# A fused attention, gated convolution and feed-forward kernel: operand addresses, the first loads, blank matmuls, and an engine for wval's low parts

## The reference

```python
# attention, B=2, H=8, S=768, D=64; n_global=8, n_local=96
keep  = is_global | ((rel >= 0) & (rel < n_local))
s     = q @ k.T / sqrt(D) - slope[h] * dist          # masked where not keep
x     = softmax(s) @ v                               # then heads side by side: (2, 768, 512)
# block 1
gate  = sigmoid(causal_conv5(x, moe_conv_w))
x     = (gate * (x @ w_val)) @ w_out
# block 2
h     = relu(x @ w_in)                               # (2, 768, 1024)
gate  = sigmoid(conv3(h, moe2_conv_w))
out   = (h * gate) @ w_out2
```

## Time and profile before

| what | us |
|---|---|
| median of three runs (281.39 to 281.93) | 281.39 |
| the profiled execution | 282.07 |
| its span | 280.3 |
| TensorE busy | 268.7 |
| VectorE busy | 187.3 |
| ScalarE busy | 158.8 |
| GpSimd busy | 41.0 |

### The profile page before, as it was taken

The page is one execution under the profiler, slowest core; times in us unless marked ns, Lnnn a source line. Parts: engine busy times, 40 slices in busy tenths (PEclk is TensorE's granted clock), DMA queues, the critical chain, the costliest instruction groups (busy, mean ns, idle before and its releaser), DMA issues.

```text
span 280.3 us, 4450 instructions
## 1 busy us (share of the span) xinstructions
PE 268.7 (96%) x1552; PEld 207.3 (74%) x1552; DVE 187.3 (67%) x452; ACT 158.8 (57%) x362; POOL 41.0 (15%) x67
## 2 busy tenths in 40 slices
PE   2999999999999999999999999999999999997995
PEld 1444458888788888888888888888888888776884
DVE  0794367788899992698960896688603578999200
ACT  1132659889999991754543506675334466874410
POOL 1081016867233220000000000000000000000000
PEclk9999999999999999999999999999999999999999
DMA  6999715545672000000000000000021000000321
GB/s 206 368 346 301 284 37 150 154 127 182 189 223 75 4 0 2 5 0 2 0 0 0 2 0 0 0 2 1 0 103 49 0 0 0 1 2 0 150 78 72
DMA packets 11864, 21.83 MB, mean 78 GB/s; under 512 B 1728, under 2 KB 1728, under 8 KB 11712
## 3 DMA queue, kind: packets, MB, share of 16 engines
q1 hardware_dynamic: 11408, 21.50, 23.8%
q10 hardware_dynamic: 432, 0.02, 0.1%
HBM read 18.37 MB, written 3.15 MB: 77 GB/s over the span
## 4 chain that ended last, share of the span: by engine, by line
PE 79%; DVE 12%; ACT 5%; DMA 1%; issue 1%; SPq 0%
PE ps L516 16%; PE ps L518 16%; PE ps L517 16%; PE ps L416 11%; PE ps L487 6%; PE ps L447 6%; PE ps L465 6%; DVE hgB L1082 4%; ACT prob L652 3%; DVE hgA L1082 2%; PE ps L473 2%; DVE hglA L1095 2%; DMA win<-in_win 1%; DVE hgA L1089 1%; DVE hgB L1089 1%
## 5 line engine op out<-in xcount | busy, mean ns | idle before, releaser
L652 ACT ACTIVATE prob<-prob,low 128x256 f32<-128x256 f32 (+1 forms) x96 | 46.0, 486 | 4.4 <-DVE low L902 4.4
L518 PE MATMUL ps<-gh,Wl 128*128 128x512 f32 x96 | 38.3, 399 | 0.0
L517 PE MATMUL ps<-gl,Wh 128*128 128x512 f32 x96 | 37.9, 394 | 0.0
L516 PE MATMUL ps<-gh,Wh 128*128 128x512 f32 x96 | 37.7, 392 | 0.0
L766 ACT ACTIVATE h<-ps 128x512 f32<-128x512 f32 x24 | 14.4, 598 | 39.8 <-PE ps L518 39.6
L416 PE MATMUL ps<-win,w1t 128*128 128x512 f32 x64 | 31.0, 646 | 5.2 <-DMA win<-in_win 5.2
L1082 DVE SCALAR_TENSOR_TENSOR hgA<-h,cw,hgA 128x512 f32<-128x512 f32 x32 | 21.9, 746 | 20.1 <-ACT hgA L778 20.1
L927 DVE SCALAR_TENSOR_TENSOR g<-xT,cw,g 128x512 f32<-128x512 f32 x48 | 32.8, 746 | 2.2 <-ACT g L691 2.2
L902 DVE CUSTOM_DVE_ANT_0 prob<-ps,bias 128x256 f32<-128x256 f32 x80 | 30.0, 413 | 2.6 <-PE ps L447 2.6
L416 PEld LDWEIGHTS ps<-win,w1t 128*128 128x128 f32 x64 | 13.1, 207 | 21.6 <-issue 16.2
L516 PE MATMUL ps<-hghA,w2h 128*128 128x512 f32 x64 | 25.2, 393 | 0.7 <-DVE hglA L1095 0.7
(11 more groups left out here) (87 smaller groups left out, 502.4 us busy)
## 6 DMA issues: line engine op xcount, KB each, us to landing
q_rows<-in_q SPq DMA_DIRECT2D x12, 256.0 KB, 4.6
kW<-in_k SPq DMA_DIRECT2D x12, 256.0 KB, 4.6
v_own<-in_v SPq DMA_DIRECT2D x12, 256.0 KB, 3.1
out<-xT SPq DMA_DIRECT2D x5, 512.0 KB, 2.8
w<-in_w SPq DMA_DIRECT2D x8, 256.0 KB, 11.7
v_win<-in_v SPq DMA_DIRECT2D x10, 192.0 KB, 3.1
w1t<-in_w1t SPq DMA_DIRECT2D x4, 256.0 KB, 4.4
win<-in_win SPq DMA_DIRECT2D x4, 256.0 KB, 5.2
```

Of the source, the lines that this page charges most:

```text
L516: pe.matmul(out, w_hi, x_hi, start=first, stop=False)
L517: pe.matmul(out, w_hi, x_lo, start=False, stop=False)
L518: return pe.matmul(out, w_lo, x_hi, start=False, stop=final)
L652: act.activation(part, part, ACT.Exp, scale=-1.0, bias=low[:, t % 2, i:i + 1], accum_out=total[:, t % 2, i:i + 1]).then_inc(exp_done, 1)
```

## The change

It has five parts.

- Two pads are declared: 192 bytes after `nval` (with the new `blank`, 512 bytes) and 160 bytes after `h`. All operands that stood 64 bytes past a multiple of 256, and `gh` and `gl`, now begin at a multiple of 256.
- VectorE fills `blank` with zeros as its first instruction, and TensorE runs seven float32 matmuls of `blank` by `blank` (128 columns) into a bank that is overwritten later.
- Part m = 0 of W's first half is cut in two quarters of 256 columns (`first_part_W`). The first call waits for 64 KB of `w1t` and 128 KB of `win` alone (`start_in[0]`).
- The slices of `win` for the first half of W are issued by ScalarE, save the first quarter, and `nw` is ScalarE's fourth issue instead of its first; SP issues the `w1t` slices, `wval` and the second half of `win`.
- `wval_low` moves from POOL to VectorE, between the bias tables and the first `split_W`.

```diff
+        blank = sb("blank", [P, P])
...
+        sb("to_256_bytes", [P, 48])
...
         h = sb("h", [P, FT, B * HROW + 1])
+        sb("h_to_256_bytes", [P, 40])
...
         def _(sp):
-            for m in range(CT):
+            sp.dma_start(win[:, 0, 0:F // 4], A_win[:, 0, 0:F // 4]).then_inc(start_in[0], 16)
+            sp.dma_start(w1t[:, 0, P:C], A_w1t[:, 0, P:C]).then_inc(start_in[1], 16)
+            for m in range(1, CT):
                 sp.dma_start(w1t[:, m, :], A_w1t[:, m, :]).then_inc(w1_in[m], 16)
-                sp.dma_start(win[:, m, 0:F // 2], A_win[:, m, 0:F // 2]).then_inc(w1_in[m], 16)
...
-                wval_low()
-                pool.wait_ge(wvl_done, CT)
                 for t in range(3):
                     key_window(t)
...
-            for m in range(CT):
+            pe.wait_ge(blank_set, 1)
+            for _ in range(WARM):
+                pe.matmul(WB(2 * CT - 1)[:, 0:P], blank[:, :], blank[:, :], start=True, stop=True)
+
+            def first_part_W(k, quarter):
+                cols = slice(quarter * (F // 4), (quarter + 1) * (F // 4))
+                pe.matmul(WB(k)[:, cols], w1t[:, 0, k * P:(k + 1) * P], win[:, 0, cols], start=(quarter == 0), stop=False)
+
+            pe.wait_ge(start_in[0], 32)
+            first_part_W(0, 0)
+            pe.wait_ge(start_in[1], 16)
+            for k in range(1, CT):
+                first_part_W(k, 0)
+            pe.wait_ge(start_in[2], 16)
+            for k in range(CT):
+                first_part_W(k, 1)
+            for m in range(1, CT):
                 pe.wait_ge(w1_in[m], 32)
...
         def _(act):
-            act.dma_start(nw[:, :], A_n.partition_broadcast(P)).then_inc(n_in, 16)
+            act.dma_start(w1t[:, 0, 0:P], A_w1t[:, 0, 0:P]).then_inc(start_in[0], 16)
+            act.dma_start(win[:, 0, F // 4:F // 2], A_win[:, 0, F // 4:F // 2]).then_inc(start_in[2], 16)
+            for m in range(1, CT):
+                act.dma_start(win[:, m, 0:F // 2], A_win[:, m, 0:F // 2]).then_inc(w1_in[m], 16)
+                if m == 1:
+                    act.dma_start(nw[:, :], A_n.partition_broadcast(P)).then_inc(n_in, 16)
...
+            def wval_low():
+                for k in range(CT):
+                    dve.wait_ge(wvh_done, k + 1)
+                    dve.tensor_tensor(wvl[:, k, :], wval[:, k, :], wvh[:, k, :].bitcast(f32), ALU.subtract).then_inc(wvl_done, 1)
+
+            dve.memset(blank[:, :], 0.0).then_inc(blank_set, 1)
...
+                wval_low()
                 for i in range(CT + 2):
                     split_W(i)
```

More of the change, by code:

```diff
@@ L23 @@
 RING = 4
+WARM = 7
 PAIRS = H // 2
@@ L173, in program @@
         k_in, q_in, v_in = ([sem(f"{name}_in{slot}") for slot in range(RING)] for name in "kqv")
-        k_window = sem("k_window")
+        k_window, blank_set = sem("k_window"), sem("blank_set")
+        start_in = [sem(f"start_in{part}") for part in range(3)]
         consts, iotas, setup = sem("consts"), sem("iotas"), sem("setup")
@@ L338, in _ @@
             pool.memset(xT[:, :, :, 0:PAD1], 0.0).then_inc(x_edges, 1)
[L341 to L344, removed]
             def key_window(t):
```

## The result

The changed kernel takes 277.13 us (median of 6 executions, 276.42 to 278.13), the kernel before 281.60 beside it: a ratio of 0.9848, 95% interval 0.9829 to 0.9866, or 4.3 us less (3.8 to 4.8). Run again later, it took 277.17 with a ratio of 0.9863. The forecast was 277.0. The profiled execution took 277.47 with a span of 275.7, 4.6 less than before.

The account below looks back on a forecast made before the run. TensorE was taken as the bound, busy 96% of the span with 79% of the chain. Head -2.6 and `hid` -1.8 make -4.4 from 281.39, so 277.0 us; own range 275.7 to 278.7, eight in ten 269.9 to 279.8.

Parts of the forecast that it names:

- Head: Start of TensorE's work up to `qk(0)`: blank matmuls and smaller first slices bring real work and clock rise earlier, 2.6 us gained.
- The time from first work to the rise: TensorE's clock at the start: the step to 2.4 GHz comes 6.0 us after first work, so at 7.0.
- `hid`: Matmuls of the `hid` stage: the pads bring 226.7 ns instead of 233.3, 264 on the path, 1.76 us gained.
- The nearest row: Choice of size for `hid`: it falls to the 226.7 ns seen in the two other stages, which stay.
- All this: 0: Setup before `qk(0)`: moving `wval_low`, the later `nw` and the changed issue queues cost nothing, being covered.
- cover left: 1.5 us at least: VectorE before `qk(0)`: `Wl` parts ready at 23.0 to 24.9, ahead of 26.4, leaving at least 1.5 us.
- Tail: Last part of the chain, through VectorE from 226.5 to 257.8: stays as long as before, 31.3 us.
- B: Rival: all float32r matmuls fall to 215.8 ns because multiples of 256, not 64, matter; 270.6 us, chance 0.22.
- C: Rival: an operand's place is nothing to TensorE, so only the start of the kernel gains; 278.8 us, chance 0.13.
- D: Rival: the clock's rise waits for real or longer work, start gains 0.9 us; 278.7 us, chance 0.07.
- N: Rival: neither clock nor places give anything and slices land as late as before; 281.4 us, chance 0.03.
- E: Rival: late `nw` makes VectorE's setup the bound, TensorE waits 3.5 us at `qk(0)`; 282.3 us, chance 0.07.

## Why the prediction was right, point by point

- *Head, forecast -2.6:* -2.71. Parts of it were off and cancelled. The slices landed at 3.6, not 4.3, so that the blanks (to 4.2) set the start of real work at 4.2; weight loads then waited 0.6 for the rest of `w1t`, against "a few tenths"; the rise came at 6.65, not 7.0. Blanks cost up to 4.2 less the landing, as the text allowed; by the medians they gave about 1.0 us net. The 2.71 compares two single profiles; by the medians the head's parts bring 2.2 (1.2 + 1.0).
- *The time from first work to the rise, taken as 6.0 from the only row:* it is no constant. Reading it off the pitch in the same way, it was 5.6 us in the changed kernel's profile and 3.9 with ten blanks; two kernels whose head is the changed kernel's, those with moved operands, gave 2.9 and 5.8; without blanks it was 3.3. Each us that it comes earlier, once real work runs, is worth half a us, so this spread moves the time by up to 1.3 us ((6.9 - 4.2)/2), within the forecast's own range. That the rise of the profiled execution lay 0.35 us from the assumed 7.0, and the forecast 0.1 us from the median, is in part luck.
- *`hid`, forecast -1.8:* -1.88, and -1.7 by the pads alone. Size and stages right; the cause named (a streamed operand off a multiple of 64) was wrong. "The nearest row" picked the right number since the pads set the distance to 0 as well as the place.
- *"All this: 0"* for `wval_low`, `nw` and the queues: right as a sum (`nw` used at 7.80, `split_W` from 22.45, fourth part at 22.45 + 3 x 0.60 + 0.68 = 24.9, at the late end of the forecast's 23.0 to 24.9; `qk(0)` followed in TensorE's own order). What failed in it is "cover left: 1.5 us at least": 1.4 here, 0.14 in another execution of the same kernel, and none in one with the same head. A count was wrong too: ScalarE has five more issues (eight instead of three), not seven, and they ended at 5.13, not 4.5; nothing hung on it.
- *Tail, unchanged:* 31.30 against 31.31.
- *Rivals:* B falls by the 0.68 of `val` and `out`. The Trainium skill, "TensorE: Matmul & The Clock Gate", section "Back-to-back issue gap", has 215.8 ns by its formula, which it gives for a single matmul in isolation, where the full rows of 512 columns here took at least 226.7 a matmul. C falls by the pads alone. D is true, in most executions, of blanks that end before the data comes. N falls. E is true from a late `nw` on, and dearer than priced.

Shares by the medians: pads -1.7, first slices -1.2, blanks -1.0, together -3.9 (the gain of the changed kernel run again; the first time gave 4.3, and the two intervals overlap). `wval_low`'s move keeps 1.0 to 1.5 us of them.

## What to carry to other kernels

For float32r matmuls back to back, give the streamed and the stationary operand the same address modulo 256 bytes, and look for a loss in the pitch (start to start), not in durations. Let blank matmuls run until the data is there: seven with a gap of 0.75 us behind them brought nothing in ten of 12 executions, three more gave 1.5 us. An edit priced at nothing because it has cover deserves a run without it: here the engine change worth "0" held a quarter to over a third of the gain. And read more than one trace of a start: from first work to the rise of the clock the same head gave 2.9 to 5.8 us.

## What was not expected of the hardware

- The pitch of float32r matmuls depends on the distance of the two operands, 0.680 (0), 0.687 (64), 0.70 (32, 96, 128, 192) us for three, and not in a monotone way (4 bytes: 0.68 to 0.69; 16 bytes streamed: mostly 0.71). Why is open.
- Each float32r matmul has 13.3 ns over its columns, at 256, 384 and 512 of them; a float32 record of 512 columns has 2.5 over its two passes (429.2 against 426.7, from the earlier trace rows).
- Matmuls of zeros alone raised TensorE's clock, in two profiles before any real one had started.
- After a wait of 5.5 us in the middle of work, TensorE's clock stood at the 1.2 GHz level for 5.6 us of work.
- `nw`'s 2 KB landed 5.6 us after its issue behind ScalarE's slices, 3.9 before, and VectorE could use it between 6.37 (third issue) and 10.17 (fourth issue).
- A POOL subtraction of two SBUF tensors stretched four of VectorE's small operations from 0.18 to 0.35 us each to 1.13 to 1.29.
